# Moving the fills of the attention's transpose banks by a step and interleaving the one-tile experts

## Chip, cores and metric

One core of a Trainium2 chip. The metric is the device time of one execution in microseconds (us). Matrix products and transposes run on TensorE (PE in the profile, PEld its weight loads), elementwise work on VectorE (DVE), ScalarE (ACT) and GpSimd (POOL), and SyncE's queue (SPq) issues most transfers.

## What is computed

The reference runs three layers behind each other on 4 x 576 tokens of width 512 (8 heads of 64): causal attention with a decay, a dense layer with 2048 hidden columns, and a layer of 8 experts in which each token goes to one.

```python
scores = scale * np.matmul(q, k.transpose(0, 1, 3, 2))
decay = cum[:, :, :, None] - cum[:, :, None, :]      # cum: cumsum of log f
attn = softmax(where(causal, -1e9, scores + decay))
x = (attn @ v)                                       # 2304 x 512
h = x @ w_in                                         # dense layer, piecewise g(h)
x = g(h) @ w_out
for e in range(8):                                   # argmax of a cosine router
    out[mask] = gate_w[mask, None] * (np.maximum(x[mask] @ w1[e], 0.0) @ w2[e])
```

## The kernel before

All float32 products are made of three passes over a high and a low part (high*high, high*low, low*high), so every operand is split: ACT (or POOL) writes the rounded high part, and the low part, the difference, comes from DVE (or POOL).

**Attention.** The 32 heads are 16 pairs. A pair has 9 steps, one for each tile of 64 query rows (of both heads, so 128 rows), and tile i has 64(i+1) keys. Each engine runs its own loop over the step number n (lines 830, 1079, 1415), and the order inside a step is the program's order on that engine. Pair p, step i stands for n = 9p + i:
- PE (1415) issues `score(n+4)`, then the transposes `turn(p, k)` of the fills that are due, then products with V: `attend_early(p)` at step 6, and for the pair before `attend_late_a` at step 2 and `attend_late_b` at step 4.
- DVE (1079) does `masked(n+3)` (decay, mask and row minimum from PSUM to `pr`), then `low(p, k)` of the fills due one step earlier on PE (L1045), then small work: `copy_late_a` at step 3, `copy_late_b` at step 5 (L1061), `denominator` at step 7 (L1035), `invert` at step 8 (L1041).
- ACT (830) does `exp(n+2)` (L799), then `high(p, k)` of the fills due one step earlier on PE (L808), and `copy_early` at step 7 (L814).

A **fill** is a set of 128x128 transposes of `pr` that fills one PSUM bank; there are 8 for each pair, numbered 0 to 7, and they alternate between two banks (`PT[k % 2]`). ACT copies a bank to `pth`, DVE subtracts to `ptl`; fill k may start when `ptl` of fill k - 2 is written. `FILL[k]` begins with the last tile that it needs, which is also the step at which it was turned: 1, 3, 5, 5, 7, 7, 8, 8. With tile 8 only, fill 7 also carries the transposed inverse row sums of the pair before.

The product of V with the first four tiles of both heads (`attend_early`, head 0 then head 1) and the product with the last five tiles of head 1 (`attend_late_b`) write the same PSUM bank PX. So `attend_early(p)` waits on `x_late_b`, which `copy_late_b(p-1)` on DVE raises:

```python
if p >= 1:
    pe.wait_ge(x_late_b, p)
head(p, 0, 0, 4, psum[:, PX, 0:4 * D], None)
head(p, 1, 0, 4, psum[:, PX, 4 * D:8 * D], early)
```

POOL splits the inputs of later pairs: for pair p `split_qk` (kh, qh, kl, ql, L577 to L584), then `split_v` (L592, L594), which waits for `attend_late_b(p-2)`, and in eight pairs `combine_x` (L632, L634), which joins pieces of x for the next layer. In the trace these eight follow the `split_v` that is released in pairs 6 to 13. SP's queue loads q, k, v, the decays and the weights, and stores x.

**Dense layer and experts.** PE then runs the dense layer in 6 groups of 384 tokens, and expert 0 densely over all tokens. A table made on the chip says which other experts have tokens; those with one tile of 128 tokens are "singles" (two in this data), at most two of them on the usual path. For single j, `up_one(j)` (16 tiles of three passes in two halves h), ACT's `relu_row`, 8 transposes (L1599), ACT's high part (L950), DVE's low part (L1287), 8 down products of three passes, and ACT's scaling of the rows (L955), which POOL scatters to `out`. `single(j)` on PE runs `up_one(j+1)`, then the transposes of j, then the down products of j; `h1h` and `h1l` have one buffer.

Of the kernel before, what the change touches and what calls it, by code (L numbers as in the profile page):

```python
# [5 lines left out]
ALU = mybir.AluOpType  # L6
ACT = mybir.ActivationFunctionType
# [13 lines left out]
def attention_moe_kernel(nc, q, k, vk, f, w_in, w_out, expert_emb, tau, w1, w2, out):  # L21
# [79 lines left out]
    def fills_of(i):  # L101
        return [k for k in range(FILLS) if FILL[k][0] == i]

    with ExitStack() as ctx:
# [134 lines left out]
        octx.close()  # L239


        rctx = ExitStack()
        sb("skipped", [P, 4 * (4 * PIECES * PIECE + 2 * KE * CH + TT * DM)], mybir.dt.uint8, rctx)
        z = sb("z", [P, NT, E], F32, rctx)
# [61 lines left out]
        def settle(engine, i):  # L306
            if not isinstance(i, int):
                engine.sem_inc(passed, 1)
# [45 lines left out]

        def tile_of(n):
            return divmod(n, NB)

        def stacked(tile, k):
            _, b, nb, i, ni = FILL[k]
# [12 lines left out]
        def _(sp):  # L372
# [177 lines left out]
            with only_if(sp, total(sp, RARE) > 0):  # L550
                singles_from(sp, 2, singles, single)
                with only_if(sp, singles > 0):
                    sp.wait_ge(up1, 2 * singles)
                    settle(sp, singles)
                full_experts(sp, expert)

# [225 lines left out]
        def _(act):  # L782
# [44 lines left out]
                act.wait_ge(wo_in_s, 16 * (f_ + 1))  # L827
                nc.scalar.copy(wouth[:, f_, :], woraw[:, f_, :]).then_inc(wo_h, 1)

            for n in range(-AHEAD, STEPS + 1):  # L830
                if 0 <= n + 2 < STEPS:
                    exp(n + 2)
                p, i = tile_of(n - 1)
                if 0 <= n - 1 < STEPS:
                    for k in fills_of(i):
                        high(p, k)
                p, i = tile_of(n)
                if i == 7 and 0 <= p < PAIRS:
                    copy_early(p)
                if p - 1 in X_LOADED and i == 1:  # L840
                    split_x(X_LOADED.index(p - 1))
                if n == 4:
                    act.wait_ge(en_turned, 1)
                    nc.scalar.copy(ent[:, :, 0:E], psum[:, RB, 0:KD * E].rearrange(
                        "p (k e) -> p k e", e=E)).then_inc(ent_h, 1)
# [76 lines left out]
                    nc.scalar.activation(rows_out[:, tt, :], psum[:, DOWN[tt], :], ACT.Copy,  # L922
                                         scale=gate[:, bass.ds(tiles[tt], 1)]).then_inc(rows_ok, 1)

            def relu_row(j):
                b = j % 2
                for h in range(2):
                    if j >= 2:
                        act.wait_ge(h1_turned, 2 * (j - 2) + h + 1)
                    act.wait_ge(up1, 2 * j + h + 1)  # L930
                    nc.scalar.activation(hrow[:, b, h, :], psum[:, UP1[b][h], :], ACT.Relu).then_inc(h1_ok, 1)

            act.wait_ge(gate_ok, 1)
            full_group(0, dense_tiles(0), False)
# [9 lines left out]
            def single(j):  # L944
                b = j % 2
                with only_if(act, singles > j + 1):
                    relu_row(j + 1)
                for h in range(2):
                    act.wait_ge(h1_turned, 2 * j + h + 1)
                    nc.scalar.copy(h1h[:, 4 * h:4 * h + 4, :], psum[:, TURN1[h], :].rearrange(  # L950
                        "p (f t) -> p f t", t=P)).then_inc(h1_h, 1)
                tile = tile1[j] if j < 2 else field(act, j, TILE, NT - 1)
                act.wait_ge(down1, j + 1)
                act.wait_ge(stored1[b], 16 * (j // 2) + 16)
                nc.scalar.activation(rows1[:, b, :], psum[:, ROW1[b], :], ACT.Copy,  # L955
                                     scale=gate[:, bass.ds(tile, 1)]).then_inc(rows1_ok, 1)

            with only_if(act, singles > 0):
                relu_row(0)
            first_two(act, singles, single)  # L960

            def expert(k, par, n, base):
# [10 lines left out]
        def _(dve):  # L973
# [105 lines left out]
            for n in range(-AHEAD, STEPS + TAIL):  # L1079
                if 0 <= n + 3 < STEPS:  # L1080
                    masked(n + 3)
                p, i = tile_of(n - 1)
                if 0 <= n - 1 < STEPS:
                    for k in fills_of(i):
                        low(p, k)
                    if i == 8 and p >= 1:
                        copy_turned(p - 1)
                p, i = tile_of(n)
                if i == 7 and 0 <= p < PAIRS:
# [193 lines left out]
            def single(j):  # L1283
                for h in range(2):
                    dve.wait_ge(h1_h, 2 * j + h + 1)
                    part = slice(4 * h, 4 * h + 4)
                    nc.vector.tensor_tensor(h1l[:, part, :], psum[:, TURN1[h], :].rearrange("p (f t) -> p f t", t=P),  # L1287
                                            h1h[:, part, :].bitcast(F32), ALU.subtract).then_inc(h1_l, 1)

            def expert(k, par, n, base):  # L1290
                for s in range(NCH):
# [16 lines left out]
        def _(pe):  # L1308
# [62 lines left out]
                if signal is not None:  # L1371
                    x.then_inc(signal, 1)

            def attend_early(p):
                pe.wait_ge(pt_l, FILLS * p + 2)
                pe.wait_ge(vsplit, p + 1)
                pe.wait_ge(ent_ok, 1)
                if p >= 1:
                    pe.wait_ge(x_late_b, p)
                head(p, 0, 0, 4, psum[:, PX, 0:4 * D], None)  # L1380
                head(p, 1, 0, 4, psum[:, PX, 4 * D:8 * D], early)

            def attend_late_a(p):
# [5 lines left out]
            def attend_late_b(p):  # L1389
                pe.wait_ge(x_early, p + 1)  # L1390
                head(p, 1, 4, 5, psum[:, PX, 0:5 * D], late_b)
# [23 lines left out]
            for n in range(-AHEAD, STEPS + TAIL):  # L1415
                if 0 <= n + AHEAD < STEPS:
                    score(n + AHEAD)
                p, i = tile_of(n)
                if 0 <= n < STEPS:
                    for k in fills_of(i):  # L1420
                        turn(p, k)
                if n in UP_EARLY:
                    up_block(UP_EARLY.index(n))
                if n == 3:
                    pe.wait_ge(en_ok, 1)
                    for m in range(KD):
                        x = nc.tensor.transpose(psum[:, RB, m * E:(m + 1) * E], emb[:, m * P:(m + 1) * P],
                                                ident[0:E, 0:E])
                    x.then_inc(en_turned, 1)
                if i == 6 and 0 <= p < PAIRS:  # L1430
                    attend_early(p)
                if i == 2 and 0 <= p - 1 < PAIRS:
                    attend_late_a(p - 1)
                if i == 4 and 0 <= p - 1 < PAIRS:
                    attend_late_b(p - 1)
                if p == PAIRS and i == 1:
                    pe.wait_ge(pt_l, FILLS * PAIRS)
                    pe.wait_ge(r_copied, PAIRS - 1)
                    turn_inverse(PAIRS - 1).then_inc(turned, 1)
# [129 lines left out]
                for tt in range(TT):  # L1569
                    out_rows(tt, par, at, first_piece, 1, hh, hl)  # L1570

            def up_one(j):
                b = j % 2
                pe.wait_ge(x1_in[b], 32 * (j // 2) + 32)
                at = slice(b * P, (b + 1) * P)
                for h in range(2):
                    if j < 2:
                        pe.wait_ge(h3_l, KE * DENSE + h + 1)
                    else:
                        pe.wait_ge(h1_ok, 2 * (j - 2) + h + 1)  # L1580
                    pe.wait_ge(p_l, CR + PIECES * (j + 1) + KD * (h + 1))
                    for m in range(KD):
                        x = three(psum[:, UP1[b][h], :], xh[:, 0, m, at], xl[:, 0, m, at],
                                  e_h[buffer_of(j)][:, KD * h + m, :], e_l[buffer_of(j)][:, KD * h + m, :],
                                  m == 0, m == KD - 1)
                    x.then_inc(up1, 1)

            def single(j):
                b = j % 2
                with only_if(pe, singles > j + 1):  # L1590
                    up_one(j + 1)
                if j == 0:
                    pe.wait_ge(rows_ok, TT * (DENSE + 1))
                if j >= 2:
                    pe.wait_ge(rows1_ok, j - 1)
                for h in range(2):
                    pe.wait_ge(h1_ok, 2 * j + h + 1)
                    for n in range(4):
                        x = nc.tensor.transpose(psum[:, TURN1[h], n * P:(n + 1) * P],  # L1599
                                                hrow[:, b, h, n * P:(n + 1) * P], ident[:])  # L1600
                    x.then_inc(h1_turned, 1)
                for f_ in range(KE):
                    pe.wait_ge(p_l, CR + PIECES * (j + 1) + 2 * KD + f_ + 1)
                    if f_ % 4 == 0:
                        pe.wait_ge(h1_l, 2 * j + f_ // 4 + 1)
                    x = three(psum[:, ROW1[b], :], h1h[:, f_, :], h1l[:, f_, :], e_h[buffer_of(j)][:, 2 * KD + f_, :],
                              e_l[buffer_of(j)][:, 2 * KD + f_, :], f_ == 0, f_ == KE - 1)
                x.then_inc(down1, 1)

            with only_if(pe, singles > 0):  # L1610
                up_one(0)
            first_two(pe, singles, single)

            def expert(k, par, n, base):
# [51 lines left out]
```

## Time and profile before

| | |
|---|---|
| median of 3 runs | 872.05 us (871.83 to 873.91) |
| the profiled execution | 873.1 us |
| its span | 871.0 us |
| PE busy | 843.6 us (97%), 5082 instructions |
| DVE, ACT, POOL busy | 418.2, 400.3, 361.5 us |
| share of PE in the chain that ended last | 91% |
| mean granted PE clock | 0.994 |
| DMA traffic | 94.59 MB, mean 109 GB/s |

A timeline row gives the start in us from the start of the span, the length, engine, line, operation, operands and shape, how many instructions are merged (x4), and in brackets how long the engine had been idle and who released it. Matmuls are pipelined, so the distance of two starts tells their cost, not the length. The stretch from about 15 to 224 us is the attention; from about 37 us on it repeats every 12.68 us, once for each pair. The experts end the span, and the one-tile experts are its last 34 us.

### The profile page before, as it was taken

How to read it: one execution, taken by the hardware profiler on the slowest of the kernel's cores; microseconds unless marked ns; L12 is line 12 of the kernel's file. 1: busy time of each engine (PE TensorE's matmuls, PEld its weight loads, DVE VectorE, ACT ScalarE, POOL GpSimd, SP SyncE). 2: the span in 40 equal slices, each digit the busy share in tenths (PEclk: the TensorE clock that was granted, in tenths of full speed). 3: DMA queues.
4: the chain of work that ended last, by engine and by line, in shares of the span. 5: the costliest groups of instructions: out<-in, count | busy, mean ns of one | idle time of the engine just before them, and what ended most of it. 6: DMA issues, size and time to landing. Idle time of an engine off the chain costs nothing.

```text
span 871.0 us, 13892 instructions
## 1 busy us (share of the span) xinstructions
PE 843.6 (97%) x5082; PEld 789.4 (91%) x5083; DVE 418.2 (48%) x1002; ACT 400.3 (46%) x915; POOL 361.5 (42%) x366
## 2 busy tenths in 40 slices
PE   7999999999999999999999999999999999999995
PEld 4888888888999999999999999999998998998984
DVE  6677888887555544444445444455535110210201
ACT  6677777777566534434444444353332111211211
POOL 5755777884565411201201121074411492010384
PEclk9899999999999999999999999999999999999999
DMA  4767788884200121021021021342223354213140
GB/s 131 223 196 229 225 260 260 251 247 112 63 1 1 46 82 53 4 100 55 28 100 55 28 100 58 118 135 68 71 91 109 99 168 133 82 40 122 37 137 26
DMA packets 66335, 94.59 MB, mean 109 GB/s; under 512 B 6662, under 2 KB 42502, under 8 KB 66256
## 3 DMA queue, kind: packets, MB, share of 16 engines
q1 hardware_dynamic: 58160, 79.43, 30.4%
q10 hardware_dynamic: 6336, 9.44, 3.0%
q0 software_dynamic: 1760, 4.72, 1.4%
q8 instruction: 43, 0.70, 0.3%
q14 instruction: 36, 0.29, 0.1%
HBM read 69.82 MB, written 24.27 MB: 108 GB/s over the span
## 4 chain that ended last, share of the span: by engine, by line
PE 91%; ACT 3%; DVE 3%; issue 1%; DMA 1%; POOL 0%; SPq 0%; ACTq 0%; POOLq 0%
PE psum L1395 24%; PE psum L1397 24%; PE psum L1396 23%; PE psum L1369 6%; PE psum L1328 5%; PE psum L1353 5%; PE psum L1334 1%; DVE ptl L1045 1%; ACT pth L808 1%; ACT xo L814 1%; ACT pr L799 1%; PE psum L1338 1%; PE psum L1470 1%; PE psum L1454 0%; PE psum L1455 0%
## 5 line engine op out<-in xcount | busy, mean ns | idle before, releaser
L1395 PE MATMUL psum<-xh,winh 128*128 128x384 f32 x384 | 129.3, 337 | 0.7 <-ACT hpos L849 0.7
L1396 PE MATMUL psum<-xl,winh 128*128 128x384 f32 x384 | 128.4, 334 | 0.0
L1397 PE MATMUL psum<-xh,winl 128*128 128x384 f32 x384 | 128.4, 334 | 0.0
L1395 PE MATMUL psum<-gh,wouth 128*128 128x384 f32 x384 | 128.4, 334 | 0.0
L1397 PE MATMUL psum<-gh,woutl 128*128 128x384 f32 x384 | 128.3, 334 | 0.0
L1396 PE MATMUL psum<-gl,wouth 128*128 128x384 f32 x384 | 128.3, 334 | 0.0
L849 ACT ACTIVATE hpos<-psum,minus 128x384 f32<-128x384 f32 x96 | 55.9, 582 | 140.8 <-DVE hclip L1071 140.6
L1074 DVE TENSOR_TENSOR g<-hpos,hsq 128x384 f32<-128x384 f32 x96 | 66.8, 696 | 111.7 <-ACT hsq L851 111.7
L632 POOL TENSOR_TENSOR xst<-xst 128x384 f32<-128x384 f32 x24 | 24.3, 1012 | 176.5 <-DMA xst<-rinv_d 176.5
L799 ACT ACTIVATE pr<-pr,mmin 128x64 f32<-128x64 f32 (+2 forms) x144 | 81.6, 567 | 30.9 <-DVE mmin L1029 30.9
L1164 DVE SCALAR_TENSOR_TENSOR hl<-psum,hh 128x384 fp32r<-128x384 f32 x48 | 26.8, 558 | 139.5 <-ACT hh L882 139.5
L1076 DVE TENSOR_TENSOR gl<-g,gh 128x384 fp32r<-128x384 f32 x96 | 63.2, 658 | 60.8 <-ACT gh L859 60.8
L1045 DVE TENSOR_TENSOR ptl<-psum,pth 128x512 fp32r<-128x512 f32 (+2 forms) x128 | 69.0, 570 | 36.0 <-ACT pth L808 35.4
L859 ACT CAST gh<-g 128x384 fp32r<-128x384 f32 x96 | 49.3, 514 | 78.3 <-DVE g L1074 78.3
L1395 PEld LDWEIGHTS psum<-xh,winh 128*128 128x128 f32 x384 | 72.1, 188 | 1.8 <-issue 1.3
L1029 DVE CUSTOM_DVE_ANT_0 pr<-psum,c 128x64 f32<-128x64 f32 (+2 forms) x144 | 67.8, 476 | 10.0 <-PE psum L1338 6.6
L1395 PEld LDWEIGHTS psum<-gh,wouth 128*128 128x128 f32 x384 | 72.1, 188 | 0.2 <-POOL woutl L646 0.2
L1353 PE MATMUL psum<-ident,pr 128*128 128x128 f32 x400 | 62.8, 284 | 9.7 <-DVE ptl L1045 9.5
L1396 PEld LDWEIGHTS psum<-xl,winh 128*128 128x128 f32 x384 | 72.1, 188 | 0.0
L1396 PEld LDWEIGHTS psum<-gl,wouth 128*128 128x128 f32 x384 | 72.1, 188 | 0.0
L1397 PEld LDWEIGHTS psum<-gh,woutl 128*128 128x128 f32 x384 | 72.1, 188 | 0.0
L1397 PEld LDWEIGHTS psum<-xh,winl 128*128 128x128 f32 x384 | 72.1, 188 | 0.0
(225 smaller groups left out, 1912.1 us busy)
## 6 DMA issues: line engine op xcount, KB each, us to landing
praw<-moe_w SPq DMA_DIRECT2D x48, 256.0 KB, 2.7
qraw<-q SPq DMA_DIRECT2D x16, 576.0 KB, 5.4
vraw<-vk SPq DMA_DIRECT2D x16, 320.0 KB, 3.0
xh<-yh_d SPq DMA_DIRECT2D x20, 256.0 KB, 4.1
xl<-yl_d SPq DMA_DIRECT2D x20, 256.0 KB, 4.4
kraw<-k SPq DMA_DIRECT2D x16, 288.0 KB, 4.3
c<-cum_d SPq DMA_DIRECT2D x32, 144.0 KB, 4.2
xa_d<-xo SPq DMA_DIRECT2D x16, 288.0 KB, 3.9
```

The lines of the kernel that those rows point to most:

```text
L799: nc.scalar.activation(region, region, ACT.Exp, bias=mmin[:, p % 2, i:i + 1], scale=-1.0, accum_out=rsum[:, p % 2, i:i + 1]).then_inc(expe ...
L849: nc.scalar.activation(hpos[:], psum[:, UP[u % 2], 0:CH], ACT.Relu, bias=minus[:, 0:1]).then_inc(up_read, 1)
L859: nc.scalar.copy(gh[:, u % NG, :], g[:]).then_inc(g_h, 1)
L1029: nc.vector.tensor_tensor_reduce(out=out_at, in0=src, in1=c_at, scale=-SCALE, scalar=LARGE, op0=ALU.add, op1=ALU.min, accum_out=mmin[:, p ...
L1045: nc.vector.tensor_tensor(stacked(ptl, k), of_bank(k), stacked(pth, k).bitcast(F32), ALU.subtract).then_inc(pt_l, 1)
L1074: nc.vector.tensor_tensor(g[:], hpos[:], hsq[:], ALU.add).then_inc(summed, 1)
L1076: nc.vector.tensor_tensor(gl[:, u % NG, :], g[:], gh[:, u % NG, :].bitcast(F32), ALU.subtract).then_inc(g_l, 1)
L1353: x = nc.tensor.transpose(psum[:, PT[k % 2], at * P:(at + 1) * P], pr[:, at_tile(i) + b * P:at_tile(i) + (b + 1) * P], ident[:])
L1369: x = nc.tensor.matmul(dst[:, (i - i0) * D:ni * D], vv[:, p % 2, b, h, :], src, start=n == 0, stop=n == len(todo) - 1)
L1395: nc.tensor.matmul(psum_at, ah, bh, start=start, stop=False)
L1396: nc.tensor.matmul(psum_at, ah, bl, start=False, stop=False)
L1397: return nc.tensor.matmul(psum_at, al, bh, start=False, stop=stop)
```

## The change

`LATER` moves fills against the step of their last tile: fill 0 one step later (step 2), fills 2 to 5 one step earlier (2 and 3 at step 4, 4 and 5 at step 6). The three loops take the fills from one function `fills_at`. On PE the fills in `BEHIND` (2 to 5) are issued behind the products with V of their step. `attend_early` is cut in two: head 0 at step 6, head 1 at step 7, and `copy_early` moves to step 8. In ACT's and DVE's loops the order inside a step stays. For the one-tile experts `h1h` and `h1l` get a second buffer in a free part of `xh` and `xl`, and PE's `single(j)` runs: first half of the next up product, the transposes of single 0, second half, the first five down products of j, the transposes of j+1, the last three down products. ACT's order follows.

```diff
+        over_x = [x[:, 1].rearrange("p k t -> p (k t)")[:, 0:KE * P].rearrange("p (f t) -> p f t", t=P)
+                  for x in (xh, xl)]
+        h1h, h1l = (h1h, over_x[0]), (h1l, over_x[1])
...
+        LATER = {0: 1, 2: -1, 3: -1, 4: -1, 5: -1}
+
+        BEHIND = (2, 3, 4, 5)
+
+        def fills_at(n):
+            at = [(n - FILL[k][0] - LATER.get(k, 0), k) for k in range(FILLS)]
+            return [(m // NB, k) for m, k in at if m % NB == 0 and 0 <= m < STEPS]
...
-            for n in range(-AHEAD, STEPS + 1):
+            for n in range(-AHEAD, STEPS + 2):
                 if 0 <= n + 2 < STEPS:
                     exp(n + 2)
-                p, i = tile_of(n - 1)
-                if 0 <= n - 1 < STEPS:
-                    for k in fills_of(i):
-                        high(p, k)
+                for p, k in fills_at(n - 1):
+                    high(p, k)
                 p, i = tile_of(n)
-                if i == 7 and 0 <= p < PAIRS:
+                if i == 8 and 0 <= p < PAIRS:
                     copy_early(p)
...
             def single(j):
                 b = j % 2
                 with only_if(act, singles > j + 1):
-                    relu_row(j + 1)
-                for h in range(2):
-                    act.wait_ge(h1_turned, 2 * j + h + 1)
-                    nc.scalar.copy(h1h[:, 4 * h:4 * h + 4, :], psum[:, TURN1[h], :].rearrange(
-                        "p (f t) -> p f t", t=P)).then_inc(h1_h, 1)
+                    relu_row(j + 1, 0)
+                if j == 0:
+                    high_one(0)
+                with only_if(act, singles > j + 1):
+                    relu_row(j + 1, 1)
+                    high_one(j + 1)
...
             for n in range(-AHEAD, STEPS + TAIL):
                 if 0 <= n + 3 < STEPS:
                     masked(n + 3)
-                p, i = tile_of(n - 1)
-                if 0 <= n - 1 < STEPS:
-                    for k in fills_of(i):
-                        low(p, k)
-                    if i == 8 and p >= 1:
+                for p, k in fills_at(n - 1):
+                    low(p, k)
+                    if k == FILLS - 1 and p >= 1:
                         copy_turned(p - 1)
...
-            def attend_early(p):
+            def attend_early_a(p):
                 pe.wait_ge(pt_l, FILLS * p + 2)
                 pe.wait_ge(vsplit, p + 1)
                 pe.wait_ge(ent_ok, 1)
                 if p >= 1:
                     pe.wait_ge(x_late_b, p)
                 head(p, 0, 0, 4, psum[:, PX, 0:4 * D], None)
+
+            def attend_early_b(p):
                 head(p, 1, 0, 4, psum[:, PX, 4 * D:8 * D], early)
...
                 p, i = tile_of(n)
-                if 0 <= n < STEPS:
-                    for k in fills_of(i):
-                        turn(p, k)
+                for p_, k in fills_at(n):
+                    if k not in BEHIND:
+                        turn(p_, k)
...
                 if i == 6 and 0 <= p < PAIRS:
-                    attend_early(p)
+                    attend_early_a(p)
+                if i == 7 and 0 <= p < PAIRS:
+                    attend_early_b(p)
                 if i == 2 and 0 <= p - 1 < PAIRS:
                     attend_late_a(p - 1)
                 if i == 4 and 0 <= p - 1 < PAIRS:
                     attend_late_b(p - 1)
+                for p_, k in fills_at(n):
+                    if k in BEHIND:
+                        turn(p_, k)
...
+            def single(j):
+                with only_if(pe, singles > j + 1):
+                    up_one(j + 1, 0)
+                if j == 0:
+                    pe.wait_ge(rows_ok, TT * (DENSE + 1))
+                    turn_one(0)
+                with only_if(pe, singles > j + 1):
+                    up_one(j + 1, 1)
+                if j >= 2:
+                    pe.wait_ge(rows1_ok, j - 1)
+                for f_ in range(KE - 3):
+                    down_one(j, f_)
+                with only_if(pe, singles > j + 1):
+                    turn_one(j + 1)
+                for f_ in range(KE - 3, KE):
+                    x = down_one(j, f_)
                 x.then_inc(down1, 1)
```

`turn_one`, `down_one` and `up_one(j, h)` hold the instructions that `single` and `up_one(j)` held; DVE's low part only takes the buffer `j % 2`. SP gets one more wait, on the path for three or more one-tile experts, which this data does not take.

## Rows read from the trace of the kernel before

**Rows 1.** Waits of PE, 37 to 212 us: total, times, longest.
```profile
PE psum L1353 <- DVE ptl L1045: 9.2, 14, 0.7
```
**Rows 2.** Timeline of PE, one pair: start us, length us, engine, line.
```profile
120.22 0.82 PE L1369 MATMUL psum<-pth,vv 128*128 128x320 f32 x5
...
123.67 0.82 PE L1369 MATMUL psum<-pth,vv 128*128 128x320 f32 x5
...
124.99 0.28 PE L1328 MATMUL psum<-kh,qh 128*128 128x64 f32 x1
...
126.39 0.42 PE L1369 MATMUL psum<-pth,vv 128*128 128x256 f32 x2
...
126.88 0.39 PE L1369 MATMUL psum<-pth,vv 128*128 128x256 f32 x2
...
129.87 0.90 PE L1353 MATMUL psum<-ident,pr 128*128 128x128 f32 x5 [0.66 <-DVE ptl L1045]
```
**Rows 3.** Timeline of DVE, the same pair.
```profile
126.66 1.02 DVE L1045 TENSOR_TENSOR ptl<-psum,pth 128x512 fp32r<-128x512 f32 x2 [0.76 <-ACT pth L808]
127.60 0.28 DVE L1029 CUSTOM_DVE_ANT_0 pr<-psum,c 128x128 f32<-128x128 f32 x1
...
128.60 0.35 DVE L1029 CUSTOM_DVE_ANT_0 pr<-psum,c 128x192 f32<-128x192 f32 x1
128.88 0.08 DVE L1029 DVE_READ_ACCUMULATOR2_ANT mmin<- 128x1 f32 x1
129.04 1.29 DVE L1045 TENSOR_TENSOR ptl<-psum,pth 128x512 fp32r<-128x512 f32 x2
130.24 0.21 DVE L1041 RECIPROCAL rinv<-rden 128x9 f32<-128x9 f32 x1
...
131.16 0.89 DVE L1045 TENSOR_TENSOR ptl<-psum,pth 128x512 fp32r<-128x512 f32 x2 [0.43 <-ACT pth L808]
```
**Rows 4.** Timeline of ACT, the same pair.
```profile
129.38 0.47 ACT L799 ACTIVATE pr<-pr,mmin 128x192 f32<-128x192 f32 x1
...
130.54 0.75 ACT L808 CAST pth<-psum 128x512 fp32r<-128x512 f32 x2 [0.60 <-PE psum L1353]
```
**Rows 5.** Timelines of DVE and PE, the last pair.
```profile
213.97 0.49 DVE L1061 COPY xo<-psum 128x320 f32<-128x320 f32 x1 [0.19 <-PE psum L1369]
...
214.60 0.42 PE L1369 MATMUL psum<-pth,vv 128*128 128x256 f32 x2
```
**Rows 6.** Timeline of POOL, the pair of rows 2, then one without combine_x.
```profile
125.32 0.72 POOL L592 TENSOR_SCALAR vv<-vraw 128x640 fp32r<-128x640 f32 x1 [2.15 <-PE psum L1369]
...
49.22 0.72 POOL L592 TENSOR_SCALAR vv<-vraw 128x640 fp32r<-128x640 f32 x1 [4.23 <-PE psum L1369]
...
51.56 0.67 POOL L577 TENSOR_SCALAR kh<-kraw 128x576 fp32r<-128x576 f32 x1
...
54.68 2.67 POOL L584 TENSOR_TENSOR ql<-qraw,qh 128x1152 fp32r<-128x1152 f32 x1
```
**Rows 7.** Timelines of POOL, DVE: a pair with combine_x, and the last but one.
```profile
102.28 0.99 POOL L632 TENSOR_TENSOR xst<-xst 128x384 f32<-128x384 f32 x1
...
102.44 0.87 DVE L1035 TENSOR_SCALAR rden<-rsum 128x9 f32<-128x9 f32 x1
...
104.96 1.17 POOL L579 TENSOR_SCALAR qh<-qraw 128x1152 fp32r<-128x1152 f32 x1
...
203.90 0.17 DVE L1035 TENSOR_SCALAR rden<-rsum 128x9 f32<-128x9 f32 x1
```
**Rows 8.** Stretch 32 to 44.6: busy time by engine, PE clock, DMA share, GB/s.
```profile
32.00:44.60 12.60, 10.67 (x85) 9.54 (x84) 8.12 (x28) 8.04 (x25) 11.77 (x9) 1.00 0.76 223
```
**Rows 9.** Timeline of PE, the one-tile experts.
```profile
848.11 1.03 PE L1599 MATMUL psum<-ident,hrow 128*128 128x128 f32 x8
850.24 0.47 PE L1395 MATMUL psum<-e_h,h1h 128*128 128x512 f32 x1 [1.10 <-DVE h1l L1287]
...
858.10 0.47 PE L1395 MATMUL psum<-e_h,h1h 128*128 128x512 f32 x1 [1.29 <-DVE h1l L1287]
```

More of the change, by code:

```diff
@@ L553, in _ @@
                     sp.wait_ge(up1, 2 * singles)
+                    settle(sp, singles)
+                    sp.wait_ge(down1, singles)
                     settle(sp, singles)
@@ L923, in full_group, with relu_row, high_one @@
                                          scale=gate[:, bass.ds(tiles[tt], 1)]).then_inc(rows_ok, 1)
-            def relu_row(j):
+            def relu_row(j, h):
                 b = j % 2
+                if j >= 2:
+                    act.wait_ge(h1_turned, 2 * (j - 2) + h + 1)
+                act.wait_ge(up1, 2 * j + h + 1)
+                nc.scalar.activation(hrow[:, b, h, :], psum[:, UP1[b][h], :], ACT.Relu).then_inc(h1_ok, 1)
+            def high_one(j):
                 for h in range(2):
[L928 to L931, printed above, removed]
+                    act.wait_ge(h1_turned, 2 * j + h + 1)
+                    nc.scalar.copy(h1h[j % 2][:, 4 * h:4 * h + 4, :], psum[:, TURN1[h], :].rearrange(
+                        "p (f t) -> p f t", t=P)).then_inc(h1_h, 1)
             act.wait_ge(gate_ok, 1)
@@ L958, in _ @@
             with only_if(act, singles > 0):
-                relu_row(0)
+                relu_row(0, 0)
+                relu_row(0, 1)
             first_two(act, singles, single)
@@ L1286, in single @@
                     part = slice(4 * h, 4 * h + 4)
-                    nc.vector.tensor_tensor(h1l[:, part, :], psum[:, TURN1[h], :].rearrange("p (f t) -> p f t", t=P),
-                                            h1h[:, part, :].bitcast(F32), ALU.subtract).then_inc(h1_l, 1)
+                    nc.vector.tensor_tensor(h1l[j % 2][:, part, :], psum[:, TURN1[h], :].rearrange("p (f t) -> p f t", t=P),
+                                            h1h[j % 2][:, part, :].bitcast(F32), ALU.subtract).then_inc(h1_l, 1)
             def expert(k, par, n, base):
@@ L1570, in full_group, with up_one, turn_one @@
                     out_rows(tt, par, at, first_piece, 1, hh, hl)
-            def up_one(j):
+            def up_one(j, h):
                 b = j % 2
-                pe.wait_ge(x1_in[b], 32 * (j // 2) + 32)
+                if h == 0:
+                    pe.wait_ge(x1_in[b], 32 * (j // 2) + 32)
                 at = slice(b * P, (b + 1) * P)
[L1576 to L1595, printed above, removed]
+                if j < 2:
+                    pe.wait_ge(h3_l, KE * DENSE + h + 1)
+                else:
+                    pe.wait_ge(h1_ok, 2 * (j - 2) + h + 1)
+                pe.wait_ge(p_l, CR + PIECES * (j + 1) + KD * (h + 1))
+                for m in range(KD):
+                    x = three(psum[:, UP1[b][h], :], xh[:, 0, m, at], xl[:, 0, m, at],
+                              e_h[buffer_of(j)][:, KD * h + m, :], e_l[buffer_of(j)][:, KD * h + m, :],
+                              m == 0, m == KD - 1)
+                x.then_inc(up1, 1)
+            def turn_one(j):
                 for h in range(2):
@@ L1599, in single, with down_one @@
                         x = nc.tensor.transpose(psum[:, TURN1[h], n * P:(n + 1) * P],
-                                                hrow[:, b, h, n * P:(n + 1) * P], ident[:])
+                                                hrow[:, j % 2, h, n * P:(n + 1) * P], ident[:])
                     x.then_inc(h1_turned, 1)
[L1602 to L1607, printed above, removed]
+            def down_one(j, f_):
+                b = j % 2
+                pe.wait_ge(p_l, CR + PIECES * (j + 1) + 2 * KD + f_ + 1)
+                if f_ % 4 == 0:
+                    pe.wait_ge(h1_l, 2 * j + f_ // 4 + 1)
+                return three(psum[:, ROW1[b], :], h1h[b][:, f_, :], h1l[b][:, f_, :],
+                             e_h[buffer_of(j)][:, 2 * KD + f_, :], e_l[buffer_of(j)][:, 2 * KD + f_, :],
+                             f_ == 0, f_ == KE - 1)
+            def single(j):
[6 more added lines that the diff above has]
+                    up_one(j + 1, 1)
+                if j >= 2:
+                    pe.wait_ge(rows1_ok, j - 1)
[5 more added lines that the diff above has]
+                    x = down_one(j, f_)
                 x.then_inc(down1, 1)
             with only_if(pe, singles > 0):
-                up_one(0)
+                up_one(0, 0)
+                up_one(0, 1)
             first_two(pe, singles, single)
```

## The prediction

> **What bounds the kernel now.** I read the waits of PE first. Over the fourteen pairs in the steady state PE waits for one thing only, `ptl` of DVE, 0.66 us each time [rows 1, 2]. Everything else in a pair is PE work back to back, so the period is PE's work plus this wait. The period is (203.90 - 102.44)/8 = 12.68 us, from the same small DVE instruction eight pairs apart [rows 7]. In the pair of [rows 2] the wait stands before the fills of tile 8, because the bank of fill 6 is released by the low part of fill 4, which was turned just before it. That is what the change spreads out. Then I read the timelines of DVE and ACT beside PE's, since a fill goes PE, ACT, DVE, PE and each engine works strictly in its program's order.
>
> **The steps of a fill, from rows.** Turn to ACT's high part: 130.54 - 129.87 = 0.67. High to DVE's low: 131.16 - 130.54 = 0.62 [rows 2 to 4]. The lows of fills 2 and 3 hold DVE 127.60 - 126.66 = 0.94, those of 4 and 5 hold it 130.24 - 129.04 = 1.20 [rows 3]. `copy_late_b` starts at 213.97 and PE's early product, which waits for it, at 214.60: 0.63 [rows 5]. So in the last pair, where no scores cover it, this wait already decides; elsewhere it is covered, since the fills' lows stand behind the copy.
>
> **Part 1, the early product gets a new wait.** Fills 2 and 3 are now turned at step 4, so their lows move to DVE's step 5, and there the loop runs the lows ahead of `copy_late_b`. Let s be the start of `attend_late_b` on PE. Its length is 124.99 - 123.67 = 1.32, then fill 2 is turned at s + 1.32. High at 1.99, low at 2.61, the copy at 2.61 + 0.94 = 3.55, the early product at 3.55 + 0.63 = s + 4.18. What PE has to cover this is fills 2 and 3 and two scores, which is the 126.39 - 124.99 = 1.40 that they take now [rows 2]; it would be ready at s + 2.72. So 1.46 us of PE are lost in every pair but the first, and the 0.66 that the change removes is less. Behind this wait stand fills 4 and 5, all later scores, and so the whole pair. Copy and early product are both in program order, so nothing can overtake them.
>
> **Part 2, the fills of tile 8 get later too.** Head 0's early product takes 126.88 - 126.39 = 0.49 [rows 2], fill 4 starts at s + 4.67, its high at 5.34, its low at 5.96. The lows of 4 and 5 now stand in DVE's step 7, ahead of `denominator` (step 7) and of the mask of the next pair's tile 2 (step 8), which is at 128.60 today, ahead of them [rows 3]. ACT has this tile's exp ahead of the high parts of fills 6 and 7. So DVE reaches `denominator` at s + 7.16, then the mask costs 128.88 + 0.08 + 0.04 - 128.60 = 0.40 to ACT, the exp 0.47 [rows 3, 4], high to low 0.62, and the lows of 6 and 7, 0.89 and 0.14 back to PE, 1.03 [rows 3]. 0.14 is 0.63 - 0.49 [rows 5]. There `attend_late_a` may start, and from it to the next s PE needs 123.67 - 120.22 = 3.45 [rows 2], with the same instructions as now. The new period is therefore 7.16 + r + 0.40 + 0.47 + 0.62 + 1.03 + 3.45 = 13.13 + r, with r the price of `denominator`.
>
> **The price of `denominator`.** It is a 128x9 instruction that takes 0.17 when POOL is idle. In the pair with `combine_x` it takes 0.87 and ends at 103.31, while POOL's instruction ends at 103.27 [rows 7]. So it waits for the end of what POOL has begun. Its place against POOL moves. POOL is released by `attend_late_b`: s + (125.32 - 123.67) = s + 1.65, and `kh` or `combine_x` follows 51.56 - 49.22 = 2.34 later, at s + 3.99 [rows 2, 6].
> - Last but one pair: POOL idle, r = 0.17, period 13.30. I take the same for pair 1.
> - The eight pairs with `combine_x`: POOL is in `qh`, which ends at 3.99 + (104.96 + 1.17 - 102.28) = s + 7.84 [rows 7]. DVE goes on at 7.87, r = 0.71, period 13.84.
> - Pairs 2 to 5: `ql` starts at 3.99 + (54.68 - 51.56) = s + 7.11 and ends at s + 9.78 [rows 6]. DVE comes at 7.16, 0.05 behind it. By this order it waits until 9.81, r = 2.65, period 15.78. The bounds of r are 0.17, if it gets in between `kl` and `ql`, and 2.65. I take the upper one, because the order of the two starts says so, though 0.05 is little after eight added durations.
>
> The Trainium skill (SBUF — State Buffer, "Who interferes with whom") says that VectorE's two-port modes and GpSimd share a port pair as an exclusive lock, held for the whole instruction by whoever issues first. The trace shows waits of this kind up to 0.87 us and none of 2.65; without such a lock r would be 0.17 everywhere and the time would be that of the rival "short chain" below.
>
> **Part 3, the rest of the attention.** The waits of fills 6 and 0 for each other's banks go; they are in the new period already. ACT's `copy_early` a step later still lies three steps before `attend_late_b` needs it: nothing. POOL's work, SP's queue and its loads get a longer pair, so they have more slack than now: nothing, and no DMA is added or moved. Fill 0 a step later costs nothing by itself, as its high part is needed only by the early product four steps on. Start and tail: pair 0 is held by its inputs, the last pair has no scores to delay. I estimate -0.5 together.
>
> **Part 4, the one-tile experts.** PE waits 1.10 and 1.29 for `h1l` there [rows 9]. From the transposes' start to the waiting product are 850.24 - 848.11 = 2.13 us. Half an up product is 12 matmuls and the last three down products 9, at 0.23 each (estimate: (858.10 - 850.24) less 1.29 and the transposes' 1.03, over 24 matmuls), so 2.8 and 2.1 us: both waits go, at most 0.1 stays. -2.4. The cover is gone only if the second single were missing.
>
> **Sum.** From the early product of pair 1 to that of pair 15 are 14 x 12.68 - 0.56 = 176.96 us now; the 0.56 is the last pair's missing scores (214.60 against 126.39 is 88.21, seven periods are 88.76) [rows 2, 5]. Then: 2 x 13.30 + 4 x 15.78 + 8 x 13.84 = 200.4, so +23.5. With -0.5 and -2.4 it is +20.6. The profiled execution took 873.1 (span 871.0), 1.05 above the median of the runs shown; 873.1 + 20.6 = 893.7, and against the median 892.65. I give **892.6**.
>
> **Rivals.**
> - *Missed slot*: the two chains hold, but `denominator` gets in ahead of `ql` in pairs 2 to 5. Four pairs at 13.30 instead of 15.78 take 9.9 off: 882.7. For it: the 0.05 us. Chance 0.28.
> - *Short chain*: only the wait of part 1 counts and POOL's hold costs nothing. 14 x 13.3 = 186.2, +9.2, in all +6.3: 878.3. Against it: the order of mask, exp and high part is fixed by the program. A little lower, 876, if ACT is quicker than the rows say. Chance 0.11.
> - *Faster*: PE does not wait for the copy, because it is done in time, and the 0.66 goes. It is decided at `x_late_b`: the change pays in a pair if the early product waits under 0.66, that is if the copy starts before s + 2.75, which is just behind fill 2's low part beginning. 14 x 0.66 and 2.9: 860. For it: it is what the reordering does to PE's banks. Against it: 3.55 by rows. Chance 0.09.
> - *Everything late*: the eight `combine_x` pairs slip too, `denominator` falling behind `qh` onto the next instruction of POOL, of 1.17 or more [rows 7]: +9 and more, 902. Chance 0.09.
> - The forecast keeps 0.43. PE's clock is no rival: in the stretch where PE was busy 10.67 of 12.60 us (85%) the granted clock was 1.00, that is 2.4 GHz [rows 8], and with 12.68 - 0.66 = 12.02 us of work the new pairs are busy at 87% or more, or 76% in the four long ones, which no row shows.
>
> **Range and chances.** 875 to 899 holds the forecast and the first two rivals, with some 3 us at either end for start, tail and the rounding of eight durations; what is left out is 0.18. 0.3% (about 2.6 us) is what a measurement of this kernel can tell from no change. Faster by more than that 0.09, within it 0.03 (the short chain with shorter steps), slower 0.88.
>
> **What would show it.** In the profile of after: a wait of PE at the V product (L1369 there) for DVE's copy `xo`, some 1.3 to 1.5 us in each pair from 2 on; the lows of fills 2 and 3 ahead of that copy; waits at the transposes or V products for `ptl` of fills 6 and 7; `denominator` of 2.7 us in pairs 2 to 5, ending with `ql`, and 0.5 to 0.7 in the `combine_x` pairs; periods of about 15.8 and 13.8; no wait for `h1l` at the end. A period under 12.68 or early products without a wait would make the forecast wrong; a period of 13.3 in pairs 2 to 5 the first rival right.

## The result, and the profile after

The changed kernel takes 897.79 us (897.52 to 898.96, 4 runs) against 872.77 in the same runs: ratio 1.0283, 95% interval 1.0263 to 1.0302. The forecast was 892.6, in a range of 875 to 899. The profiled execution took 898.96. Here and below, executions over 1.5% above the fastest of their kernel are left out of the ratios (one of e7 at 1669.31, one of e9 at 873.84, one of before at 4490.35 beside e5 to e8).

The page: span, busy time, granted clock of PE in 40 slices, and the engines' share of the chain that ended last.

```profile
span 896.8 us, 13898 instructions
PE 852.5 (95%) x5082; PEld 796.9 (89%) x5083; DVE 428.1 (48%) x1002; ACT 398.0 (44%) x915; POOL 359.4 (40%) x366
...
PEclk9899899999999999999999999999999999999999
...
PE 83%; DVE 8%; ACT 4%; issue 3%; DMA 1%; DVEq 0%; POOL 0%; SPq 0%; POOLq 0%; ACTq 0%
```

PE has the same 5082 instructions as before, and the 25.8 us of span are time in which it waits or runs slower. DVE's share of the chain was 3% and is 8%. The second and the fifth digit of the clock row are 8; in before only the second is.

PE's waits from 37 to 240 us, the counterpart of [rows 1]:

```profile
PE psum L1388 <- DVE xo L1082: 15.8, 14, 1.3
PE psum L1372 <- DVE ptl L1066: 7.1, 18, 1.0
PE psum L1347 <- DVE mmin L1050: 4.7, 4, 1.2
```

The first row is the new wait of part 1: the early product for the copy of the product before it, 14 times, 15.8 us (six of 1.29, seven of 1.05, one of 0.77). The one row of before, 9.2 us on the transposes, has become 7.1 in other places: 5.4 at fill 0, which waits for the low part of fill 6, and 1.7 at fill 3, which waits for that of fill 1. Another 4.7 us are new ahead of the score of tile 6, which waits for the mask of tile 2.

One pair (pair 3 to 4), first PE, then DVE, ACT and POOL:

```profile
62.26 0.83 PE L1388 MATMUL psum<-pth,vv 128*128 128x320 f32 x5
...
63.58 0.88 PE L1372 MATMUL psum<-ident,pr 128*128 128x128 f32 x6
...
66.46 0.42 PE L1388 MATMUL psum<-pth,vv 128*128 128x256 f32 x2 [1.29 <-DVE xo L1082]
...
72.36 0.47 PE L1347 MATMUL psum<-kh,qh 128*128 128x448 f32 x1 [1.17 <-DVE mmin L1050]
...
74.23 0.41 PE L1372 MATMUL psum<-ident,pr 128*128 128x128 f32 x2 [0.94 <-DVE ptl L1066]
...
75.06 1.41 PE L1388 MATMUL psum<-ptl,vv 128*128 128x320 f32 x5
76.29 0.77 PE L1347 MATMUL psum<-kh,qh 128*128 128x512 f32 x1
```

```profile
64.89 1.02 DVE L1066 TENSOR_TENSOR ptl<-psum,pth 128x512 fp32r<-128x512 f32 x2 [1.29 <-ACT pth L824]
65.83 0.48 DVE L1082 COPY xo<-psum 128x320 f32<-128x320 f32 x1
...
68.22 1.29 DVE L1066 TENSOR_TENSOR ptl<-psum,pth 128x512 fp32r<-128x512 f32 x2 [1.55 <-ACT pth L824]
69.42 2.62 DVE L1056 TENSOR_SCALAR rden<-rsum 128x9 f32<-128x9 f32 x1
71.96 0.34 DVE L1050 CUSTOM_DVE_ANT_0 pr<-psum,c 128x192 f32<-128x192 f32 x1
```

```profile
72.34 0.46 ACT L815 ACTIVATE pr<-pr,mmin 128x192 f32<-128x192 f32 x1 [2.81 <-DVE mmin L1050]
```

```profile
68.00 1.42 POOL L597 TENSOR_TENSOR kl<-kraw,kh 128x576 fp32r<-128x576 f32 x1
69.38 2.64 POOL L600 TENSOR_TENSOR ql<-qraw,qh 128x1152 fp32r<-128x1152 f32 x1
```

With s = 62.26 the forecast's offsets can be read off: fill 2 at +1.32 (said 1.32), its low part at +2.63 (2.61), the copy at +3.57 (3.55), the early product at +4.20 (4.18), `denominator` at +7.16 (7.16), the mask of tile 2 at +9.70 (9.81), its exp at +10.08 (10.21). `ql` starts at 69.38 and `denominator` at 69.42, 0.04 behind it; it ends at 72.04, `ql` at 72.02. In the pairs before and after (53.82 against 53.78, 86.59 against 86.53, 103.76 against 103.73) it loses the same way. In pairs 7 to 10 and 12 to 14 the early product comes at +4.38 or +4.39: fill 3 waits 0.24 there first, and 1.05 is left of the wait for the copy.

The last rows of PE are something the forecast excluded: from 75.06 on the merged five products take 1.41 us where five such products take 0.82 in [rows 2]. That is the clock. Pair by pair, from one early product to the next (busy PE, PEld, DVE, ACT, POOL, then the granted clock, DMA share, GB/s):

```profile
50.86:66.46 15.60, 12.19 (x93) 10.90 (x94) 11.53 (x32) 9.27 (x27) 8.02 (x7) 1.00 0.55 169
66.46:83.63 17.17, 13.76 (x94) 12.17 (x94) 11.66 (x32) 9.17 (x27) 8.02 (x7) 0.90 0.50 153
117.97:131.88 13.91, 12.26 (x94) 10.83 (x94) 11.12 (x33) 9.57 (x28) 10.21 (x9) 1.00 0.71 213
173.04:187.68 14.64, 13.35 (x93) 12.28 (x94) 10.13 (x33) 9.89 (x28) 9.82 (x9) 0.88 0.75 239
```

Pair 2 takes 15.60 at a clock of 1.00; pairs 3, 4 and 5 take 17.17 each, with a mean of 0.90 (0.90 on all three), and pair 10 takes 14.64 at 0.88. The others with `combine_x` take 13.70 to 13.91, pair 1 13.17 and pair 14 13.25. The lower clock itself, 0.50 of full speed or 1.2 GHz, stands in short stretches, in pair 3, pair 10 and the last pair:

```profile
75.25:78.25 3.00, 3.00 (x11) 2.38 (x12) 1.69 (x7) 1.84 (x7) 0.00 (x0) 0.50 0.71 238
174.25:177.25 3.00, 3.00 (x17) 2.87 (x16) 1.91 (x6) 2.16 (x6) 3.00 (x4) 0.50 0.89 289
242.50:245.50 3.00, 3.00 (x15) 3.00 (x15) 0.66 (x1) 1.01 (x2) 2.83 (x4) 0.50 0.64 149
```

Ahead of the second and the third, PE had just waited for the copy:

```profile
173.04 0.42 PE L1388 MATMUL psum<-pth,vv 128*128 128x256 f32 x2 [1.05 <-DVE xo L1082]
242.27 0.62 PE L1388 MATMUL psum<-pth,vv 128*128 128x256 f32 x2 [2.00 <-DVE xo L1082]
```

At the end of the span, PE at the one-tile experts, the counterpart of [rows 9]:

```profile
874.11 1.03 PE L1618 MATMUL psum<-ident,hrow 128*128 128x128 f32 x8
...
877.73 0.39 PE L1416 MATMUL psum<-e_h,h1h 128*128 128x512 f32 x1
...
881.13 1.03 PE L1618 MATMUL psum<-ident,hrow 128*128 128x128 f32 x8
881.92 0.48 PE L1416 MATMUL psum<-e_h,h1h 128*128 128x512 f32 x1
```

No product here has a wait in brackets any more. The transposes of the first single are followed by half an up product and then by `h1h` products 0.68 apart; those of the second by a down product after 0.79.

### The profile page after: what moved, and what is told of

Its sections match the earlier page's. It is cut to its first block, busy times and chain, and to the rows that moved or that the text cites. A ratio compares the mean times of both kernels' runs of the same rounds, so it can differ in the third digit from the quotient of the medians.

```text
span 896.8 us, 13898 instructions
## 1 busy us (share of the span) xinstructions
PE 852.5 (95%) x5082; PEld 796.9 (89%) x5083; DVE 428.1 (48%) x1002; ACT 398.0 (44%) x915; POOL 359.4 (40%) x366
## 4 chain that ended last, share of the span: by engine, by line
PE 83%; DVE 8%; ACT 4%; issue 3%; DMA 1%; DVEq 0%; POOL 0%; SPq 0%; POOLq 0%; ACTq 0%
PE psum L1416 23%; PE psum L1418 23%; PE psum L1417 23%; PE psum L1388 4%; PE psum L1372 4%; PE psum L1347 3%; DVE ptl L1066 3%; ACT pth L824 2%; DVE rden L1056 1%; ACT pr L815 1%; DVE xl L1087 1%; DVE pr L1050 1%; DVE xo L1082 1%; PE psum L1353 1%; PE psum L1496 1%
## 5 line engine op out<-in xcount | busy, mean ns | idle before, releaser
L1372 PE MATMUL psum<-ident,pr 128*128 128x128 f32 x400 | 64.9, 290 | 7.9 <-DVE ptl L1066 7.1
L824 ACT CAST pth<-psum 128x512 fp32r<-128x512 f32 (+2 forms) x128 | 57.8, 487 | 31.6 <-PE psum L1372 31.3
```

What stands on the lines that cost most here:

```text
L824: nc.scalar.copy(stacked(pth, k), of_bank(k)).then_inc(pt_h, 1)
L1372: x = nc.tensor.transpose(psum[:, PT[k % 2], at * P:(at + 1) * P], pr[:, at_tile(i) + b * P:at_tile(i) + (b + 1) * P], ident[:])
```

## The experiments

Every ratio is to the kernel before, timed beside it.

**e1, the experts alone.**

```diff
-        LATER = {0: 1, 2: -1, 3: -1, 4: -1, 5: -1}
-        BEHIND = (2, 3, 4, 5)
+        LATER = {}
+        BEHIND = ()
```

Besides, `attend_early_b` goes back to step 6 and `copy_early` to step 7.

> The attention's order of before (LATER empty, BEHIND empty, both heads of the early product at step 6), the one-tile experts interleaved as in the change. My theory: the two waits for h1l of 1.10 and 1.29 us go, 872.8 - 2.4 = 870.4 us, ratio 0.997, and the attention's period stays 12.68. Rival, that the gain of the interleaving is given back by a new wait on the transposes of the second single or at ACT: 872.8, ratio 1.000.

Measured: 869.76 us, ratio 0.9966 (0.9953 to 0.9979), that is -3.0 us, and the expected -2.4 lies inside the interval. The period is 12.68 in all pairs, and no wait for `h1l` is left. Part 4 is right, and all the loss is the attention's.

**e2, the copy ahead of the lows.** One call in DVE's loop moves:

```diff
+                p, i = tile_of(n)
+                if i == 5 and 0 <= p - 1 < PAIRS:
+                    copy_late_b(p - 1)
                 for p, k in fills_at(n - 1):
                     low(p, k)
...
-                if i == 5 and 0 <= p - 1 < PAIRS:
-                    copy_late_b(p - 1)
```

> The change, with one edit in DVE's loop: copy_late_b stands ahead of the low parts of fills 2 and 3 in step 5. My theory (the early product waits because the copy is queued behind these lows): the wait of 1.29 us at head 0's product goes in every pair, denominator comes at s + 5.7 instead of s + 7.16 and meets shorter instructions of POOL, so it costs 0.1 to 0.4; periods 11.8 to 12.0, or 13.1 in pairs 2 to 5 if it just misses the gap behind qh; 858 to 866 us. Rival, that the early product waits for the product before it and not for the copy's place, or that the low parts of fills 2 and 3 coming later cost as much: periods stay over 13, 885 to 898 us.

Measured: 865.37 us, ratio 0.9932 (0.9909 to 0.9955), 32 us under the change. No wait for `xo` is left; periods are 13.0 to 13.1 in pairs 2 to 5, 11.94 to 12.44 in the `combine_x` pairs. The 13.0 is the case "just misses the gap": `denominator` waits for `kl`, as DVE and POOL show (pair 3):

```profile
65.10 1.21 DVE L1056 TENSOR_SCALAR rden<-rsum 128x9 f32<-128x9 f32 x1
```

```profile
64.87 1.42 POOL L597 TENSOR_TENSOR kl<-kraw,kh 128x576 fp32r<-128x576 f32 x1
```

It ends at 66.31, `kl` at 66.29. So part 1 stands: the place of one copy of 0.49 us decides the sign of the change. Not all of the 32 us are the wait for the copy. The steps behind it come earlier too, so `denominator` takes 1.21 instead of 2.62 in pairs 2 to 5 and `xl` (split_x) 0.74 to 1.23 instead of mostly 1.65 in the `combine_x` pairs, and the clock stays at 1.00.

**e3, no denominator.** The addition of 1e-9 to the row sums is left out: `denominator` is no longer called, and what waited for it waits for the row sums or for the reciprocal.

```diff
-                    act.wait_ge(den_ok, p - 1)
+                    act.wait_ge(inv_ok, p - 1)
...
-                dve.wait_ge(den_ok, p + 1)
+                dve.wait_ge(exped, NB * (p + 1))
...
-                nc.vector.reciprocal(rinv[:, p % 2, 0:NB], rden[:, p % 2, :]).then_inc(inv_ok, 1)
+                nc.vector.reciprocal(rinv[:, p % 2, 0:NB], rsum[:, p % 2, :]).then_inc(inv_ok, 1)
...
-                if i == 7 and 0 <= p < PAIRS:
-                    denominator(p)
```

> The change without the denominator instruction: the reciprocal is taken of the row sums directly, so the addition of 1e-9 is left out, and ACT's exp waits for the reciprocal in its place. My theory (2.62 us of DVE in pairs 2 to 5 are a wait for POOL's ql, and the gaps that it leaves on PE bring the lower granted clock of 0.90): the periods of 15.6 and 17.17 become 13.1 to 13.2, those with combine_x 13.1 to 13.5, the granted clock of each pair is 1.00, and 876 to 881 us result. Rival, that pairs 2 to 5 are long because the mask of tile 2 comes late for another reason: periods stay over 15, 890 us or more.

Measured: 882.06 us, ratio 1.0099 (1.0084 to 1.0114). A stretch of the length of one pair without `combine_x` and one with:

```profile
50.00:63.10 13.10, 11.81 (x95) 10.74 (x95) 9.04 (x30) 9.26 (x28) 8.04 (x6) 1.00 0.66 201
120.00:133.70 13.70, 12.38 (x95) 10.77 (x95) 10.90 (x32) 9.54 (x29) 10.00 (x9) 1.00 0.75 236
```

Periods are 13.11 to 13.13 in pairs 1 to 5, as 13.13 + r with r = 0 said, and the clock is 1.00 in every pair. The `combine_x` pairs stay at 13.7 (one at 14.2): DVE's other instruction that waits for POOL, `xl` (0.74 us in before), takes 2.03 to 2.52 here. That is why the time is 1 us above the expected range.

**e4, the gap filled.** Four products whose result nothing uses, in pairs 3 to 6:

```diff
+                if n in (3 * NB + 2, 4 * NB + 2, 5 * NB + 2, 6 * NB + 2):
+                    pe.wait_ge(x_late_a, n // NB - 1)
+                    for _ in range(4):
+                        nc.tensor.matmul(psum[:, PY, :].rearrange("p (a b) -> p a b", a=4), ident_b[:],
+                                         ident_b[:].unsqueeze(1).to_broadcast([P, 4, P]), start=True, stop=True)
```

> The change, with four extra bf16 products (128x512) into PSUM bank PY ahead of the score of tile 6 in pairs 3 to 6, where PE sits idle for 1.17 us in the change. Their result is used by nothing. My theory (the periods of 17.17 are 15.6 plus 1.57 from the stretch at 1.2 GHz that follows the two gaps of 1.17 and 0.94): the granted clock of these pairs goes from 0.90 to 1.00, the three periods of 17.17 become 15.6 to 15.8, and the time falls by 4 to 5 us to 893 or 894. Rival, that the clock is not what makes them long: the extra products cost nothing or up to 0.1 us each where the gap does not hold them, 898 to 899.

Measured: 893.8 us (891.53 to 896.46), ratio 1.0231 (1.0214 to 1.0247). The profiled execution is the slowest of the four. Two of the pairs, and the products in the gap:

```profile
82.00:97.60 15.60, 13.05 (x100) 11.15 (x98) 11.52 (x31) 9.28 (x28) 8.04 (x7) 1.00 0.55 169
97.60:113.20 15.60, 13.06 (x100) 11.16 (x99) 11.50 (x31) 9.29 (x28) 8.04 (x7) 1.00 0.71 208
```

```profile
73.02 1.03 PE L1440 MATMUL psum<-ident_b 128*128 128x512 bf16 x4
74.38 0.47 PE L1347 MATMUL psum<-kh,qh 128*128 128x448 f32 x1 [0.33 <-DVE mmin L1050]
```

The wait of 1.17 is 0.33, the clock 1.00, the periods 15.59 to 15.61 instead of 17.17. More work on PE made the kernel faster by 4.0 us, of the 3 x 1.57 = 4.7 of these pairs; pair 13 takes 15.02 at a clock of 0.89 here, and pair 10 no longer has its drop. The 1.57 us in a pair are the clock's. The executions without a trace agree: the mean granted clock is 0.991 to 0.995 in the four of e4, 0.985 to 0.987 in the four of the change. This run also has a `combine_x` pair at full clock, pair 8, in which `xl` takes only 0.54, and `denominator` 0.16: from early product to early product it takes 13.14 instead of 13.7.

**e7, fills 2 and 3 alone.** Before's attention with `LATER = {2: -1, 3: -1}` and `BEHIND = (2, 3)`.

> The attention of before with fills 2 and 3 alone moved to step 4, behind the product with V, everything else of the attention in its old place (fill 0 too), the experts interleaved. My theory (the early product waits 1.3 to 1.46 us for the copy behind the lows): periods of 14.1, up to 14.7 in the pairs with combine_x, where split_x may wait for POOL's ql; 890 to 897 us, so nearly all of the change's loss comes from these two fills. Rival, that it takes all four fills together (the mask of tile 2 behind the lows of 4 and 5): 870 to 880.

Measured: 891.6 us (ratio 1.0197, 1.0166 to 1.0228). PE's waits:

```profile
PE psum L1388 <- DVE xo L1082: 18.8, 14, 2.0
PE psum L1372 <- DVE ptl L1066: 7.2, 11, 0.7
```

The period is 14.15 to 14.16 in eleven pairs (14.1 expected) and 15.0 in three, at a clock of 0.89. In two of these three the clock falls about 1 us behind a wait of 1.29, which the other pairs have too; ahead of the first one PE had waited only 0.83 and 0.22. Moving two fills into the step of the copy brings some three quarters of the loss of all four (from the experts' 0.9966 to 1.0197, against 1.0283), not nearly all as expected; the long `xl` of 1.84 to 1.88 in most `combine_x` pairs does not lengthen them here.

**e6, fills 4 and 5 alone (with fill 0).** `LATER = {0: 1, 4: -1, 5: -1}`, `BEHIND = (4, 5)`.

> The change with fills 2 and 3 left at step 5 (LATER holds 0, 4 and 5, BEHIND 4 and 5). My theory: the early product of head 0 finds the copy done, so no wait for it; fills 4 and 5 are turned at s + 3.2, denominator comes at s + 5.7, just ahead of the end of POOL's qh at s + 5.8 in pairs 2 to 5; periods of 11.8 there and 12.0 in the pairs with combine_x, 858 to 861 us. If denominator misses that gap, it waits for kl to s + 7.15 and pairs 2 to 5 take 13.1: 865. Rival, that fills 4 and 5 ahead of denominator and the mask of tile 2 lose by themselves: over 872.

Measured: 881.26 us (ratio 1.0088, 1.0064 to 1.0113), a miss by 20. PE in pair 3, then DVE's `denominator`:

```profile
73.94 0.85 PE L1372 MATMUL psum<-ident,pr 128*128 128x128 f32 x6
...
76.07 1.06 PE L1372 MATMUL psum<-ident,pr 128*128 128x128 f32 x8 [0.46 <-DVE ptl L1066]
```

```profile
78.56 0.87 DVE L1056 TENSOR_SCALAR rden<-rsum 128x9 f32<-128x9 f32 x1
```

I had left out the bank. Fill 4 uses that of fill 2, so it can't start before fill 2's low part is done, 76.07 - 73.94 = 2.13 us after it, the same 2.13 that before has between fills 4 and 6 (129.87 less 127.74, the start of fill 4 there). It starts at s + 3.8, not s + 3.2, `denominator` comes 0.6 later than I had it, misses `qh` and waits 0.87 for `kl`. Periods are 13.0 in pairs 2 to 5 and 13.7 in the `combine_x` pairs (11.8 and 12.0 expected), so most of the miss is in the latter, eight times 1.7. There `denominator` takes only 0.35 to 0.49, and `xl` 1.66 (2.77 once). So fills 4 and 5 alone gain nothing here, while e2, with all four moved, gains.

**e8, e6 without the denominator** (the addition of 1e-9 is left out).

> e6 without the denominator instruction (the addition of 1e-9 is left out). My theory: all pairs run at PE's own work, 11.7 to 11.8, 856 to 858 us. Rival, that the mask, exp and high part of the next chain hold the period at 12.0 or more whatever denominator costs: as e6.

Measured: 873.69 us (867.85 to 876.53, 10 runs), ratio 0.9992 (0.9964 to 1.002). Neither holds as a whole: periods of 12.27 in pairs 2 to 6, with 0.46 us of the bank's wait, 12.3 to 12.5 in the next four, where `xl` takes 0.54 to 0.86, but 13.7 in pairs 11 to 13, where it takes 1.9 to 2.7, and 17.56 in pair 1, where PE was idle for 2.21 us and the clock was then 0.81.

**e5 and e10, copy first and no denominator** (e2 with e3's edit; the addition of 1e-9 is left out).

> e2 (copy_late_b ahead of the lows) without the denominator instruction (the addition of 1e-9 is left out, the reciprocal is taken of the row sums directly). In e2 pairs 2 to 5 still take 13.0, with 1.21 us for denominator. My theory: these pairs fall to 11.8 to 12.0 like the eight with combine_x, 865.4 - 4 to 6 us, 859 to 861. Rival, that PE and ACT alone set 13.0 there: 865.

> e5 once more in five rounds (the addition of 1e-9 is left out), because e9's executions spread from 861 to 874 us, with DVE's xl (split_x) of 2.7 us in some pairs, where it comes behind the start of POOL's ql. My theory: in e5 xl comes during kl, ahead of ql, so the executions stay together at 858 to 862 us and xl under 1.5 us. Rival, that every version with short pairs spreads, e5 having been lucky in four executions: executions up to 870 and a median of 863 or more.

Measured: 859.7 us (858.25 to 861.01), ratio 0.9836 (0.9809 to 0.9864), and again 859.73 (858.16 to 860.1), ratio 0.985 (0.983 to 0.987). PE's waits from 37 to 240 us in the second:

```profile
PE psum L1415 <- ACT hpos L863: 0.7, 2, 0.5
PE psum L1371 <- DVE ptl L1066: 0.7, 1, 0.7
```

Periods are 11.92 to 11.99, but for two of 12.1 in e5 and three of 12.2 to 12.7 in e10, and `xl` takes 0.80 to 1.50. This is PE's own work (11.86 of 11.93 us), and e10 beats the kernel before by 1.5% and the change by 4.2%. Since the maximum of a row is subtracted ahead of exp, a row sum is at least 1 and 1e-9 is under half a unit in its last place in float32.

**e9, denominator kept, elsewhere.** e2 with `denominator(p - 1)` at step 4 and `invert(p - 1)` at step 6 of the next pair.

> e2 with nothing left out: copy_late_b ahead of the lows, and denominator kept whole but moved from step 7 to step 4 of the next pair, the reciprocal from step 8 to step 6 of the next pair (the last pair keeps its places). There POOL is through with ql in the pairs without combine_x, so denominator should take 0.17, and up to about 1 us in the others, where DVE has slack. My theory (what costs in e2 is only denominator's hold in front of the mask of tile 2): periods of 11.9 to 12.1 in all pairs, 859 to 862 us, as e5. Rival, that e5 gained from having one DVE instruction fewer and not from its place: between e2 and e5, 863 to 865.

Measured: 867.6 us, but 860.9 to 873.84 over seven executions, ratio 0.9915 (0.9875 to 0.9955). The profiled one has nine periods of 11.92 to 11.95, two of 13.7 and three of 12.7 to 12.9. POOL and DVE in one of 13.7, and then DVE and POOL in e10:

```profile
115.85 2.69 POOL L600 TENSOR_TENSOR ql<-qraw,qh 128x1152 fp32r<-128x1152 f32 x1
```

```profile
116.23 2.72 DVE L1087 TENSOR_TENSOR xl<-xst,xh 128x384 fp32r<-128x384 f32 x1
```

```profile
113.19 0.80 DVE L1087 TENSOR_TENSOR xl<-xst,xh 128x384 fp32r<-128x384 f32 x1
```

```profile
113.53 3.00 POOL L600 TENSOR_TENSOR ql<-qraw,qh 128x1152 fp32r<-128x1152 f32 x1
```

In e9 `xl` comes 0.38 us behind the start of `ql` and ends 0.41 us behind its end (118.95 and 118.54). In e10 it comes during `kl`, is done 0.8 us later, again 0.41 behind the end of `kl` (113.58), and it is `ql` that is pushed (3.00 instead of 2.66). In pair 8 of e9 `xl` comes 0.11 behind the reported start of `ql` and still gets in: it takes 0.54, and `ql` 3.20. Which of the two happens in e9 differs from pair to pair and, by the spread of the times, from execution to execution; the other executions have no trace here, so the last is argued, not shown. In the profiled execution the `combine_x` pairs, from early product to early product, follow `xl`: 13.7 with 2.7 us of it, 12.8 with 1.4 to 1.6, 11.8 to 12.0 with 0.54 to 1.06. The theory of the expectation holds for `denominator` (0.16 to 0.61 after the first pair), the time lies in neither range.

## Why the prediction was right, and where it was not

- **Part 1** held to 0.02 us in pairs 2 to 6 and 11: early product at s + 4.20, 1.48 behind the s + 2.72 at which it could be ready (said 1.46); the profile counts 1.29 of it as idle. In seven others the same 1.29 are split into 0.24 and 1.05. e2 and e7 show the cause from both sides.
- **Part 2** held: e3's 13.11 against 13.13.
- **The price of `denominator`** held on a margin of 0.04 us (said 0.05): 2.62 in four pairs, the rival "missed slot" did not occur. In the `combine_x` pairs it took 0.23 to 0.68 (said 0.71). The Trainium skill's rule of the exclusive port pair (SBUF — State Buffer, "Who interferes with whom") is borne out up to 2.62 us, three times what the trace of before had; its further sentence, that an instruction of VectorE with two SBUF inputs contends with GpSimd's reads, is what `xl` shows, 2.72 us in e9.
- **A sum that is right for partly other reasons.** The `combine_x` pairs took 13.70 to 13.91 (said 13.84), and `xl` waits for `ql` there, 1.65 us instead of 0.74. e3 has them at 13.7 without any `denominator`, and pair 8 of e4, whose `xl` does not wait, takes 13.14, so it is `xl` that holds them, and not `denominator` alone. The change moves `split_x` against POOL too, and I had priced only the small instruction.
- **The step that failed** is the sentence in the rivals that PE's clock is no rival. The row it rested on had 85% of PE busy with its idle time elsewhere; the change has 12.19 of 15.60, 78%, in pair 2, with 1.17 and 0.94 us idle within 3.1 us (71.19 to 74.23 in pair 3). Three pairs of 1.57 and one of about 0.9 are 5.6 us, which the sum has nowhere. From the early product of pair 1 to that of pair 15 it was 204.6 (said 200.4): 5.6 is the clock, and the other terms were 1.4 too high together. So 4.1 of the 5.2 us between forecast and measurement lie up to pair 15, and without the terms that were too high the miss would have been larger.
- **Part 4** held: -3.0 in e1, -2.4 said.
- **Start and tail** were taken at -0.5; of the 25.8 us of span, +27.6 up to pair 15 and -2.4 at the end leave +0.6. This too is the clock: from 242.3 us on it is at 0.50, and from the last early product to the end of the span the change takes 654.5 us, against 653.0 to 653.6 in e1, e3 and e7, where the clock does not fall there. That is the other 1.1 of the 5.2.

## What to carry to other kernels

To move a step on one engine, list what stands behind it in the program's order of every engine that follows it. Here a copy of 0.49 us slipped behind 0.94 us of other work, and its place alone decided between +2.8% and -0.7%. Small DVE instructions next to a busy POOL are priced by what POOL has just begun, so write down both starts; if the margin is some 0.05 us, take the instruction out of the way rather than trust the order.

## What the runs showed of the hardware

- A DVE instruction that takes 0.17 beside an idle POOL [rows 7] took 2.62, and one of 0.74 in before took 2.72. The first ended within 0.05 us of the end of POOL's instruction, the second 0.41 behind it. If DVE's is already waiting when one instruction of POOL ends, it gets in ahead of the next, and POOL's is longer instead (`ql` 3.00 against 2.66). The order of two reported starts is not the whole rule: `denominator` lost all eight times that it came 0.03 to 0.06 behind `ql` (the change and e4), while `xl` got in at 0.06 to 0.14 (e4, e8, e9) and lost from 0.32 on (e6, e8, e9).
- The granted clock of PE fell to 1.2 GHz for part of a pair after two idle stretches of 1.17 and 0.94 us close together, in three pairs in a row, but not in the first pair with the same gaps (15.60 at 1.00). It also fell about 1 us behind a single wait of 1.05 us (pair 10; pair 13 of e4) or 1.29 us (two pairs of e7), and right behind one of 2.00 us (the last pair). Most waits of these lengths had no fall behind them (none from pair 1 on in e3, with six of 1.29, eight of about 1 and one of 2.00), and what picks the pair stays open. Filling 0.84 us of the first gap with useless products kept the clock at 2.4 GHz in all four pairs with both gaps.
